# Forming the x operands of a seven-product layer on GpSimd instead of VectorE, in a fused attention and two-MoE kernel

## The reference

```python
# 1. clustered attention, 2 batches x 8 heads, 768 rows, head size 64 -> x (1536 x 512)
# 2. MoE with capacity: 8 experts, 192 tokens each, chosen greedily by the largest gate logits
for e in range(8):
    mask = assigned == e
    h = np.maximum(x[mask] @ w1[e], 0.0)
    out[mask] = h @ w2[e]
# 3. dense MoE over 4 experts on all 1536 rows
p = domain_probs / (domain_probs.sum(-1, keepdims=True) + 1e-09)
for e in range(4):
    h = np.maximum(x @ w1[e], 0.0)
    out += p[:, e:e + 1] * (h @ w2[e])
```

## Time and profile before

| | us |
|---|---|
| median of 3 runs | 1086.81 |
| lowest and highest run | 1083.71, 1090.9 |
| the profiled execution, device time | 1086.81 |
| the profiled execution, span of the trace | 1085.0 |
| TensorE busy in the span | 1024.5 |
| VectorE, ScalarE, GpSimd busy | 623.0, 506.3, 441.9 |

### The profile page before, as it was taken

The page is one execution under the profiler, slowest core; times in us unless marked ns, Lnnn a source line. Parts: engine busy times, 40 slices in busy tenths (PEclk is TensorE's granted clock), DMA queues, the critical chain, the costliest instruction groups (busy, mean ns, idle before and its releaser), DMA issues.

```text
span 1085.0 us, 18093 instructions
## 1 busy us (share of the span) xinstructions
PE 1024.5 (94%) x6458; PEld 934.0 (86%) x6458; DVE 623.0 (57%) x1332; ACT 506.3 (47%) x1007; POOL 441.9 (41%) x363
## 2 busy tenths in 40 slices
PE   3999999999987799999999999999999999999996
PEld 3888888888877789999899988899999888999995
DVE  2788888888835535555223444555559445555542
ACT  3798888888851233333643333233324332333230
POOL 7032323233100111111266685665566756665542
PEclk9999999999997599999999999999999999999999
DMA  3323232332120724445962212211222322212201
GB/s 97 81 74 82 73 80 75 78 81 71 29 118 14 249 79 170 171 171 171 252 167 78 68 49 78 79 61 60 75 78 70 106 78 79 65 59 72 78 1 59
DMA packets 75170, 99.61 MB, mean 92 GB/s; under 512 B 5728, under 2 KB 44640, under 8 KB 74848
## 3 DMA queue, kind: packets, MB, share of 16 engines
q1 hardware_dynamic: 72400, 92.39, 28.0%
q0 software_dynamic: 2704, 6.33, 1.9%
HBM read 79.80 MB, written 6.32 MB: 79 GB/s over the span
## 4 chain that ended last, share of the span: by engine, by line
PE 83%; ACT 9%; DVE 3%; issue 3%; DMA 1%; POOL 1%; ACTq 0%; SPq 0%; DVEq 0%; POOLq 0%
PE ps_y L1416 9%; PE ps_y L1417 9%; PE ps_y L1415 9%; PE ps_h L1442 8%; PE ps_y L1457 7%; PE ps_h L1417 6%; PE ps_h L1415 6%; PE ps_h L1416 6%; PE ps_t L1320 4%; PE ps_s L1307 3%; ACT p_hi L707 2%; PE ps_s L1308 2%; PE ps_m L1281 2%; PE ps_o L1334 2%; PE ps_o L1335 2%
## 5 line engine op out<-in xcount | busy, mean ns | idle before, releaser
L560 POOL TENSOR_TENSOR w_lo<-w_sum,w_hi 128x1792 fp32r<-128x1792 f32 x32 | 129.8, 4079 | 62.8 <-ACT w_hi L782 62.8
L1417 PE MATMUL ps_y<-b_lo,h_hi 128*128 128x512 f32 x384 | 149.7, 390 | 0.0
L1416 PE MATMUL ps_y<-b_hi,h_lo 128*128 128x512 f32 x384 | 149.7, 390 | 0.0
L1415 PE MATMUL ps_y<-b_hi,h_hi 128*128 128x512 f32 x384 | 149.4, 389 | 0.0
L1231 DVE SCALAR_TENSOR_TENSOR Y<-ps_y,mix_n,Y 128x512 f32<-128x512 f32 x84 | 63.0, 750 | 134.5 <-PE ps_y L1417 134.4
L1415 PE MATMUL ps_h<-x_hi,w_hi 128*128 128x384 f32 x384 | 128.6, 335 | 0.0
L1417 PE MATMUL ps_h<-x_lo,w_hi 128*128 128x384 f32 x384 | 128.5, 335 | 0.0
L1416 PE MATMUL ps_h<-x_hi,w_lo 128*128 128x384 f32 x384 | 128.4, 334 | 0.0
L566 POOL TENSOR_TENSOR b_lo<-b_raw,b_hi 128x2048 fp32r<-128x2048 f32 x16 | 74.0, 4626 | 114.4 <-ACT b_hi L789 113.7
L975 DVE TENSOR_TENSOR p_lo<-ps_t,p_hi 128x384 fp32r<-128x384 f32 x192 | 101.6, 549 | 22.5 <-ACT p_hi L707 22.3
L581 POOL DMA_INDIRECT rows_in<-x_rows,ids x16 | 16.7, 1044 | 222.9 <-DVE ids L1083 212.7
(11 more groups left out here) (201 smaller groups left out, 2343.0 us busy)
## 6 DMA issues: line engine op xcount, KB each, us to landing
w_sum<-in_moe_w_dram SPq DMA_DIRECT2D x64, 256.0 KB, 3.2
b_raw<-in_moe_w_dram SPq DMA_DIRECT2D x16, 1024.0 KB
raw_a<-in_moe_w_dram SPq DMA_DIRECT2D x8, 1024.0 KB, 6.5
raw_b<-in_moe_w_dram SPq DMA_DIRECT2D x8, 1024.0 KB
odd_a<-in_moe_w_dram SPq DMA_DIRECT2D x8, 1024.0 KB, 7.5
odd_b<-in_moe_w_dram SPq DMA_DIRECT2D x8, 1024.0 KB
khhT<-kqT SPq DMA_DIRECT2D x32, 192.0 KB, 3.1
raw_k<-in_k_dram SPq DMA_DIRECT2D x16, 192.0 KB, 2.4
```

Of the source, the lines that this page charges most:

```text
L560: g.tensor_tensor(w_lo[t][:], w_sum[t][:, 1:8], w_hi[t][:].bitcast(F32), ALU.subtract).then_inc(wlo_done[t], 1)
L1415: t_.matmul(dst, w_hi, x_hi, start=first, stop=False)
L1416: t_.matmul(dst, w_lo, x_hi, start=False, stop=False)
L1417: return t_.matmul(dst, w_hi, x_lo, start=False, stop=last)
```

## The change

The four block sums of group 0 move from VectorE to GpSimd, between `ids_by_tile(0, ...)` and `expert_rows(6)`. The seven low parts of group 1 move from VectorE to GpSimd: five between `w_low(8, 0)` and `w_low(8, 1)`, two behind `w_low(8, 1)`. ScalarE makes `w_hi` of (8, 0) ahead of the seven high parts instead of behind them. VectorE, which no longer orders these reads by its own program order, waits for `xlo_done` 14 before the outputs of J = 8. The low parts of group 0 stay on VectorE.

```diff
--- before.py
+++ after.py
@@ -529,18 +529,23 @@
                 split_head(h, 0)
                 split_head(h, 1)
 
-            def later_x_sums():
-
-                b11, b12 = xs[:, 1, 0:2, 0, :], xs[:, 1, 0:2, 1, :]
-                b21, b22 = xs[:, 1, 2:4, 0, :], xs[:, 1, 2:4, 1, :]
-                pool.wait_ge(xlo_done, 7)
-                pool.wait_ge(y_taken, 2 * E)
+            def x_sums(gr):
+
+                b11, b12 = xs[:, gr, 0:2, 0, :], xs[:, gr, 0:2, 1, :]
+                b21, b22 = xs[:, gr, 2:4, 0, :], xs[:, gr, 2:4, 1, :]
+                at_least(pool, xlo_done, 7 * gr)
+                pool.wait_ge(y_taken, 2 * (E // 2) * (gr + 1))
                 g.tensor_tensor(x_sum[0][:], b12, b11, ALU.subtract).then_inc(xsum_step, 1)
-                pool.wait_ge(xsum_step, 5)
+                pool.wait_ge(xsum_step, 4 * gr + 1)
                 g.tensor_tensor(x_sum[1][:], b22, x_sum[0][:], ALU.subtract).then_inc(xsum_step, 1)
                 g.tensor_tensor(b12, b22, b12, ALU.subtract).then_inc(xsum_step, 1)
-                pool.wait_ge(xsum_step, 6)
+                pool.wait_ge(xsum_step, 4 * gr + 2)
                 g.tensor_tensor(x_sum[2][:], x_sum[1][:], b21, ALU.subtract).then_inc(xsum_step, 1)
+
+            def x_low(gr, k):
+
+                pool.wait_ge(xhi_done, 7 * gr + k + 1)
+                g.tensor_tensor(x_lo[:, k], x_part(gr, k), x_hi[:, k].bitcast(F32), ALU.subtract).then_inc(xlo_done, 1)
 
             def w_sums(J, t):
 
@@ -607,6 +612,7 @@
                 keep_ids(n)
             pool.wait_ge(ids_out[0], 16 * EARLY)
             ids_by_tile(0, 0, T_EARLY)
+            x_sums(0)
             for n in range(EARLY, E):
                 expert_rows(n)
                 keep_ids(n)
@@ -626,12 +632,20 @@
             for J in range(NJ):
                 b_low(J)
                 if J == 1:
-                    later_x_sums()
+                    x_sums(1)
                 if J + 1 < NJ:
                     for t in range(2):
                         w_sums(J + 1, t)
-                    for t in range(2):
-                        w_low(J + 1, t)
+                    if J + 1 == NJ // 2:
+                        w_low(J + 1, 0)
+                        for k in range(5):
+                            x_low(1, k)
+                        w_low(J + 1, 1)
+                        for k in range(5, 7):
+                            x_low(1, k)
+                    else:
+                        for t in range(2):
+                            w_low(J + 1, t)
                 if J == NJ // 2:
                     rows_out(0)
             rows_out(1)
@@ -885,10 +899,10 @@
                 keep_first(2 * J + 1)
                 slice_highs(2 * J + 1)
                 if J + 1 < NJ:
+                    w_high(J + 1, 0)
                     if J + 1 == NJ // 2:
                         for k in range(7):
                             x_high(1, k)
-                    w_high(J + 1, 0)
                     w_high(J + 1, 1)
 
 
@@ -1160,27 +1174,9 @@
             token_ids(E - 2)
             token_ids(E - 1)
 
-            def first_x_sums():
-
-                b11, b12 = xs[:, 0, 0:2, 0, :], xs[:, 0, 0:2, 1, :]
-                b21, b22 = xs[:, 0, 2:4, 0, :], xs[:, 0, 2:4, 1, :]
-                dve.wait_ge(y_taken, 2 * (E // 2))
-                v_.tensor_tensor(x_sum[0][:], b12, b11, ALU.subtract).then_inc(xsum_step, 1)
-                dve.wait_ge(xsum_step, 1)
-                v_.tensor_tensor(x_sum[1][:], b22, x_sum[0][:], ALU.subtract).then_inc(xsum_step, 1)
-                v_.tensor_tensor(b12, b22, b12, ALU.subtract).then_inc(xsum_step, 1)
-                dve.wait_ge(xsum_step, 2)
-                v_.tensor_tensor(x_sum[2][:], x_sum[1][:], b21, ALU.subtract).then_inc(xsum_step, 1)
-
-            def x_low(gr, k):
-
-                dve.wait_ge(xhi_done, 7 * gr + k + 1)
-                at_least(dve, m_full, 7 * (4 * E2 * gr - 1) + k + 1)
-                v_.tensor_tensor(x_lo[:, k], x_part(gr, k), x_hi[:, k].bitcast(F32), ALU.subtract).then_inc(xlo_done, 1)
-
-            first_x_sums()
             for k in range(7):
-                x_low(0, k)
+                dve.wait_ge(xhi_done, k + 1)
+                v_.tensor_tensor(x_lo[:, k], x_part(0, k), x_hi[:, k].bitcast(F32), ALU.subtract).then_inc(xlo_done, 1)
 
             def product_sum(s_, last, out_, in0, in1, op=ALU.add):
 
@@ -1216,12 +1212,10 @@
                 product_sum(s_, 7, at[4], c_167[t][:], at[4], ALU.subtract)
                 d_low(s_, 4, bank[4], 0, 1)
 
-            def outputs(J, lows):
+            def outputs(J):
 
                 gr, ex = J // (2 * E2), J // 2 % E2
                 for q in range(TPB):
-                    for k in lows[q + 1:q + 2] if q else lows[0:2]:
-                        x_low(1, k)
                     dve.wait_ge(o_full, TPB * J + q + 1)
                     t = out_tile(gr, q)
                     if J % (2 * E2) == 0:
@@ -1235,7 +1229,9 @@
             for J in range(NJ):
                 for t in range(2):
                     slice_sums(2 * J + t)
-                outputs(J, range(7) if J + 1 == NJ // 2 else ())
+                if J == NJ // 2:
+                    dve.wait_ge(xlo_done, 14)
+                outputs(J)
 
 
         @block.tensor
```

## The result

| | before | after |
|---|---|---|
| median, us | 1086.81 | 1098.61 |
| lowest and highest run | 1083.71, 1090.9 | 1092.06, 1105.75 |
| the profiled execution, device time | 1086.81 | 1099.44 |
| its span | 1085.0 | 1097.7 |
| VectorE, GpSimd busy in the span | 623.0, 441.9 | 612.9, 460.6 |

The ratio is 1.0107, with a 95% interval of 1.007 to 1.0143: the change costs 11.8 us at the medians. The forecast was 1092.9 us with a range to 1098: the side was right, the size half of it, and the outcome lies 0.6 us above the range and just over the 1% that was given 3 chances in 100.

What follows compares the result with a forecast made beforehand. TensorE was taken to bound the kernel, carrying 83% of the chain of waits. Part 1's 4.4 us and part 2's 1.65 us made 6.05 us on 1086.81, so 1092.9 us, range 1086 to 1098.

Steps and rivals of the forecast that it cites:

- the gains of nothing: Instructions taken off VectorE, four sums and seven in stage 3, gain 0 because TensorE did not wait for them.
- Rival 4: Whole kernel: the freed VectorE gives something, at best 1084.8 us; chance 0.03.
- part 2: Stage 3, J = 8: low parts k = 5 and 6 from GpSimd reach TensorE late, 0.9 and 0.75 us; +1.65 us.
- part 1: End of phase 6: group 0's sums on GpSimd hold VectorE's small instructions by turns, delaying ScalarE's chain; +4.4 us.
- rival 1: End of phase 6: the sums don't meet VectorE's chain, only part 2 counts; 1088.5 us, chance 0.22.
- rival 2: End of phase 6: tensor_scalar (over, same) is held as well; 5.2 + 1.65 us, 1093.7 us, chance 0.10.
- rival 3: TensorE's granted clock falls under 1.00 after 520 us; 1.8 us allowed in the range, chance 0.09.

Runs made afterwards that it cites:

- lows_only: Kernel before with only the seven low parts of group 1 on GpSimd, ScalarE's new order and VectorE's new wait: ratio 1.0016, median 1089.18 us.
- sums_clock_kept: sums_only plus 80 small unread matmuls on TensorE ahead of the ranks of phase 6: ratio 1.0050 against the kernel before, median 1091.63 us.
- sums_only: Kernel before with only the four block sums of group 0 moved to GpSimd, at the change's early place: ratio 1.0073, median 1095.01 us.
- before_fed: Kernel before plus 8 and 20 unread matmuls ahead of the token matmuls of phases 6 and 7: ratio 0.9994, median 1085.89 us.
- after_again: The changed kernel, unaltered, measured again against the kernel before: ratio 1.0108, median 1097.61 us.
- after_late_sums: Changed kernel with the four sums of group 0 on GpSimd behind expert 6's gather: ratio 1.0000 against the kernel before, median 1087.66 us.
- seven_lows_first: after_late_sums with all seven low parts of group 1 ahead of w_low(8, 1): one run, 1089.0 us.
- two_sums_early: sums_only with two sums left at the early place and two behind expert 6's gather: ratio 1.0028 against the kernel before, median 1089.65 us.
- late_sums_only: Kernel before with only the four sums of group 0 moved to GpSimd, behind expert 6's gather: ratio 0.9989, median 1086.24 us.
- writes_early: late_sums_only plus four GpSimd memsets at the early place: one run, 1094.46 us against 1086.82 for the kernel before.
- sums_fed: sums_clock_kept plus 8 and 20 unread matmuls ahead of the token matmuls of phases 6 and 7: ratio 1.0031 against the kernel before, median 1091.47 us.
- late_sums_fed: late_sums_only plus 8 and 20 unread matmuls ahead of the token matmuls of phases 6 and 7: ratio 0.9978 against the kernel before, median 1084.72 us.

## Why the prediction was right or wrong

**Right: what bounds, and the gains of nothing.** The stretch of 31 us that holds the lows, windows after (11.23 us later than in the earlier trace rows, as stage 3 is):

```profile
823.53:854.53 31.00, 29.77 (x148) 26.27 (x147) 14.44 (x26) 14.17 (x19) 27.50 (x14) 1.00 0.15 40
```

VectorE's busy time fell from 28.28 to 14.44 us, GpSimd's rose from 19.09 to 27.50 us, and TensorE, which had no idle time to win back (31.00 us busy of 31.00), has 1.23 us of it now: the two waits for `x_lo`. Rival 4 is out.

**Right: part 2, +1.65 us.** The sixth low part was to be 0.9 us late and is 0.94; the seventh another 0.75 and is 0.74, by starts (the recorded idle times are 0.78 and 0.46, for records of matmuls overlap: here 0.33 us long and 0.17 from start to start). Another tenth goes at the restarts, where the next matmul starts 0.28 us on in place of 0.17, so it is 1.79 us in all, and 1.7 us by the timed lows_only. The spacing of 1.80 us, from the sums of the same size, was right, `b_lo(8)` stayed hidden (it ends at 852.23 us, and the second layer starts at 856.13), and VectorE's new wait cost nothing: the last low part is there at 847.65 us, and the first output of J = 8, at 859.16, waited for TensorE. This was a sum over a queue with all its terms in rows.

**Right: the mechanism of part 1.** GpSimd's instructions and VectorE's took turns, whole instruction by whole instruction, and instructions of 12 elements were held (1.32 to 1.84 us for 0.22 or 0.23) as one of 768 was (4.52 us for 0.96). That was carried over from the earlier trace rows, and rival 1, that small instructions slip through, is out. GpSimd's queue order cost nothing either: behind the sums it waited 12.76 us for the ids of expert 6.

**Wrong, and small: which instructions are held.** The step took `chosen_in`, `chosen_in`, the scan and `e_sum`, because the rows showed only instructions with two SBUF inputs held. In fact the holds begin at `over`, so rival 2 was the course of things: `over` and `same` took 1.32 and 1.77 us for 0.23. The prediction gave it 0.10. The price of this step was nearly right all the same. Without the clock, `slot_far` follows `slot` by 0.29 us (9.37 and 9.66 us behind `found` in sums_clock_kept), so the hold of the changed kernel is 8.47 + 0.29 - 3.81 = 4.95 us on ScalarE's chain, where the sum had 4.4 and rival 2 had 5.2. In part this is luck: the first sum began 0.07 us ahead of `found` and not 0.57, and the four took 7.22 us and not the 7.86 that the step gave them with VectorE's turns in between, and these two misses nearly cancel. Where the sums start 0.9 us later against `found`, as in sums_only, it is 0.9 us more; that depends on the landing of the ids, and the prediction took the one landing that it had.

**Wrong, and large: the clock.** The step that failed is in part 1: "TensorE, 3.1 us late, reaches both slot_hot ahead of ScalarE still, and waits", and with it the sum, which put the clock at nothing. By that step the 0.67 us of idle time ahead of the first `slot_hot` grow by 4.4 - 3.1 = 1.3 to 2.0 us, and slower matmuls could hide in them. The time to hide in was smaller: TensorE's ranks are 4.95 us late (7.54 us behind `found` in place of 2.59) and not 3.1, just as late as ScalarE's chain without the clock. So all that was left is the 0.67 us of idle time ahead of the tokens; it is there again in sums_clock_kept, and gone in the changed kernel. The 28 matmuls take 7.59 - 4.80 = 2.79 us longer, so TensorE by its own order is 2.1 us late beyond the hold. And the two engines do not run beside each other either. Timeline of ScalarE after:

```profile
525.68 0.33 ACT L827 ACTIVATE h<-ps_h 128x192 f32<-128x192 f32 x1 [6.79 <-PE ps_h L1438]
525.91 1.48 ACT L833 ACTIVATE slot_far<-steps,slot 128x192 bf16<-128x192 f32 x4
528.25 0.33 ACT L827 ACTIVATE h<-ps_h 128x192 f32<-128x192 f32 x1 [0.86 <-PE ps_h L1438]
...
530.35 0.33 ACT L827 ACTIVATE h<-ps_h 128x192 f32<-128x192 f32 x1 [0.40 <-PE ps_h L1438]
```

Between each four `slot_far` ScalarE's program has an activation `h` that needs TensorE's next products. At a clock of 1.00 they are ready (no idle time between the groups in before or in sums_clock_kept). At 0.53 the first `slot_far`, queued behind such an `h`, starts 1.03 us behind `slot` instead of 0.29, and ScalarE waits 0.86 and 0.40 us more in between. The products are part of ScalarE's chain, which is as late as TensorE's own: `slot_hot` ends at 534.37 us and TensorE is through with its work at 534.35. So beyond those 0.67 us ScalarE left no time to hide the fall in. The token matmuls of phase 6 are 18.01 - 10.85 = 7.16 us late against 4.95: the first fall costs 2.2 of its 2.8 us. The second fall costs 5.18 - 3.50 = 1.68 us. The 1.35 us of idle time ahead of it left the clock at 1.00 in the one profile that the prediction had; it does not always, and the sum has nothing for it.

**The sum, put right.** Hold 4.95, first fall 2.21, second fall 1.67, one late wait near stage 3 0.49: 9.32 of the 9.33 us. That wait is for ScalarE's `h`, recorded as 0.22 us; by starts it is 0.27 us more, as it is in before_fed (0.79 and 1.06). Timeline of TensorE after:

```profile
583.97 8.39 PE L1453 MATMUL ps_y<-h,odd_b 128*128 128x192 f32 x50 [0.22 <-ACT h L827]
```

With part 2, 1.79, that is 11.1 us in place of 6.05, and the medians say 11.8. Of the 5 us missed the clock is nearly 4. That is the account of one profile: whether the second fall is the change's doing is not shown (see Open).

**Wrong: rivals as alternatives.** Rival 2 and the clock, rival 3, are one event: a longer hold makes a longer idle time (4.77 us, not 3.1), and behind 4.65 us and more the clock fell in all three profiles, behind 1.15 to 1.64 us at this place in none. Early in the attention the clock of the kernel before is at 0.50 behind 1.95 us. What 3.1 us would have done at this place, no run shows, and more idle time did not mean a longer fall (5.70 us: 28 matmuls in 7.04 us; 4.65 us: 7.72 us). The prediction gave the two 0.10 and 0.09 as if they excluded each other. Its range did add them up, but with 1.8 us for the clock: 1098 less 1092.9 is 5.1 us, of which 2.5 are scatter and 0.8 rival 2's (1093.7 less 1092.9). No run shows these 1.8 us, an estimate of the author's; the profile shows 3.9. Together, 5.2 + 1.65 + 3.9 = 10.8 us, they are what happened; with the same 2.5 us of scatter added, the range would have had to reach to 1100.

**Open.** What decides the second fall. Of the eleven profiles in which TensorE waits 1.35 us there with nothing in between, the 20 matmuls behind the wait were slow in six (after, after_again, sums_only, after_late_sums, seven_lows_first: 1.7 us; sums_clock_kept: 3.0 us) and at full clock in five others (before, lows_only, two_sums_early, late_sums_only, writes_early), with sums early and late in both groups. It may account for part of the scatter between executions of one kernel; no run timed that.

## What to carry to other kernels

Before work is given to GpSimd, list what VectorE does in those microseconds: if it is a chain of small dependent instructions on the critical path, each can be held as long as the GpSimd instruction beside it runs, however small it is (four of 12 elements lost 1.09 to 1.62 us each beside sums of 1.80 to 1.82 us here, 5.74 in all), and the same work at another place can be free (15 us later it cost nothing here, 0.9989 and 1.0000). Then ask what TensorE does while that chain is late, and count its clock as part of the same event, not as a separate risk (here 0.53 behind 4.77 us of idle time, 2.2 us of the 9.3). And a slack between two engines counts only if neither waits for the other inside it: look for the instruction in the middle of the chain that does.

## What the runs showed of the hardware

- Beside GpSimd's `tensor_tensor` of 128x768, a `tensor_scalar` of 12 float32 elements for each partition, one SBUF tensor input, took 1.21 to 1.32 us (`over`) and 1.77 or 1.78 us (`same`) for 0.23, and 2.15 to 2.26 us in the three profiles where it began while GpSimd still issued a DMA. A `scalar_tensor_tensor` of 12, `chosen_in`, took 1.84 or 1.85 and 1.72 or 1.73 us for 0.22 or 0.23, in five profiles.
- Beside a GpSimd memset of 128x2304 (writes_early, one profile) the `tensor_scalar` instructions took 0.73 and 2.01 us for 0.23, and 1.31 us for 0.22 (`closing`, 8 elements). In the middle of a memset a `chosen_in` took 0.23 us, the scan 0.21 us, and `e_num`, a `tensor_scalar` of a single element with an int32 output, 0.15 us (517.88 us), all as without one. Two long records there, of a `chosen_in` (1.87 us) and of `e_sum` (1.18 us), end with those of `same` and `closing` ahead of them.
- GpSimd lost nothing by the turns: its four sums ran from 516.34 to 523.56 us, 7.22 us, where those of group 1 took 7.32 us.
- A TensorE idle for 4.65 to 5.70 us went to a granted clock of 0.50 to 0.54 over the 5 us behind it in all three profiles that had that, and 28 matmuls took 7.04 to 7.72 us for 4.80. Idle for 1.15 to 1.64 us at the same place, in four others (sums_clock_kept, sums_fed, two_sums_early, writes_early), the 28 matmuls behind it took 4.80 us, at 1.00; in the first two of these the wait came behind 80 small matmuls. Idle for 1.35 us at a later place, ahead of 24 matmuls of two columns, it had a lower clock behind the wait in six of eleven profiles (20 matmuls in 5.18 or 6.54 us for 3.50), and idle for 1.86 us near stage 3 in the one profile that had that (0.71 from 580 to 585 us).
- With small matmuls that nobody reads in its waits, TensorE kept the clock at 1.00 there: 80 in sums_clock_kept (510 to 530 us), 80, 8 and 20 in sums_fed (510 to 578 us), 8 and 20 in before_fed and late_sums_fed (515 to 560 us). The 8 and 20 alone cost before nothing that can be measured (0.9994).
